# Two heads' last 64 keys turned and multiplied as one block, and a pair's outputs gathered in one bank

## The reference, cut to what matters

```python
# batch 4, 8 heads, 576 rows, 64 channels a head
scores = scale * np.matmul(q, k.transpose(0, 1, 3, 2))
thresh = np.max(scores, axis=-1, keepdims=True) - tau
scores = np.where(scores >= thresh, scores, -1000000000.0)
scores = scores - np.max(scores, axis=-1, keepdims=True)
attn = np.exp(scores)
attn = attn / (np.sum(attn, axis=-1, keepdims=True) + 1e-09)
attn_out = np.matmul(attn, v)
# then a gated layer on the heads side by side: k = relu(xk @ w_k), v = k*k @ w_v, times sigmoid(xr @ w_r);
# then a two-dimensional Fourier transform, a normalisation and relu(un @ w_ch1) @ w_ch2
```

## Time and profile before

| | us |
|---|---|
| median of 3 runs | 1071.75 (1071.11 to 1073.01) |
| profiled execution, device time | 1072.66 |
| its span | 1070.9 |
| PE busy in the span | 1051.8 |
| DVE busy | 577.4 |
| ACT busy | 513.3 |
| POOL busy | 414.1 |

### The profile page before, as it was taken

The page is one execution under the profiler, slowest core; times in us unless marked ns, Lnnn a source line. Parts: engine busy times, 40 slices in busy tenths (PEclk is TensorE's granted clock), DMA queues, the critical chain, the costliest instruction groups (busy, mean ns, idle before and its releaser), DMA issues.

```text
span 1070.9 us, 18505 instructions
## 1 busy us (share of the span) xinstructions
PE 1051.8 (98%) x7088; PEld 1000.9 (93%) x7088; DVE 577.4 (54%) x1119; ACT 513.3 (48%) x1252; POOL 414.1 (39%) x362
## 2 busy tenths in 40 slices
PE   7999899999999999999999999999999999999998
PEld 6999899999999999999999999888888888888998
DVE  6888885467965467865455788434214114123211
ACT  5999775646875646875746653121111111111110
POOL 4878784343664343664312345441111111111000
PEclk9999999999999999999999999999999999999999
DMA  8636111024211024211013217200100100100000
GB/s 242 192 89 194 36 49 49 11 80 126 87 41 56 4 80 126 94 34 36 2 45 142 79 50 289 96 1 36 36 1 27 45 1 8 63 2 1 36 1 34
DMA packets 39992, 70.10 MB, mean 65 GB/s; under 512 B 4320, under 2 KB 21088, under 8 KB 39392
## 3 DMA queue, kind: packets, MB, share of 16 engines
q1 hardware_dynamic: 39600, 68.59, 20.2%
q10 hardware_dynamic: 304, 0.33, 0.1%
HBM read 56.50 MB, written 12.41 MB: 64 GB/s over the span
## 4 chain that ended last, share of the span: by engine, by line
PE 89%; POOL 4%; ACT 3%; DVE 2%; issue 1%; DMA 0%; SPq 0%; DVEq 0%; ACTq 0%; POOLq 0%
PE PB L807 22%; PE PB L809 21%; PE PB L808 21%; PE PB L867 11%; PE PB L834 7%; PE PB L850 6%; ACT probsT L1121 1%; ACT exps L1112 1%; POOL wkl L673 1%; DVE probs L1392 1%; POOL cs_lo L685 0%; POOL k_lo L664 0%; DVE neg_s L1381 0%; POOL q_hl L657 0%; DMA k_raw<-kT_dram 0%
## 5 line engine op out<-in xcount | busy, mean ns | idle before, releaser
L1340 ACT ACTIVATE h_hi<-PB 128x464 fp32r<-128x464 f32 (+1 forms) x80 | 44.5, 556 | 329.8 <-PE PB L809 329.8
L1615 DVE SCALAR_TENSOR_TENSOR h_lo<-PB,h_hi 128x464 fp32r<-128x464 f32 (+1 forms) x80 | 51.0, 638 | 256.7 <-ACT h_hi L1340 256.7
L867 PE MATMUL PB<-v_sb,probsT 128*128 128x64 f32 (+1 forms) x1440 | 177.8, 271 | 0.0
L867 PEld LDWEIGHTS PB<-v_sb,probsT 128*128 128x128 f32 x1440 | 172.6, 192 | 0.0
L1392 DVE SCALAR_TENSOR_TENSOR probs<-neg_s,thresh,exps 128x576 f32<-128x576 f32 x144 | 160.0, 1111 | 2.7 <-ACT exps L1112 2.3
L1121 ACT ACTIVATE probsT<-PB 128x384 f32<-128x384 f32 (+1 forms) x288 | 110.6, 439 | 78.1 <-PE PB L850 77.0
L1381 DVE TENSOR_SCALAR_CACHE_REDUCE neg_s<-PB,taus 128x576 f32<-128x576 f32 x144 | 117.0, 813 | 47.9 <-PE PB L834 44.6
L809 PE MATMUL PB<-un_h,w1l 128*128 128x464 f32 (+1 forms) x320 | 118.8, 371 | 0.0
L808 PE MATMUL PB<-h_lo,w2h 128*128 128x464 f32 (+1 forms) x320 | 118.8, 371 | 0.0
L807 PE MATMUL PB<-h_hi,w2h 128*128 128x464 f32 (+1 forms) x320 | 118.8, 371 | 0.0
L809 PE MATMUL PB<-h_hi,w2l 128*128 128x464 f32 (+1 forms) x320 | 118.8, 371 | 0.0
(11 more groups left out here) (195 smaller groups left out, 2359.7 us busy)
## 6 DMA issues: line engine op xcount, KB each, us to landing
q_raw<-qT_dram SPq DMA_DIRECT2D x62, 160.0 KB, 3.1
k_raw<-kT_dram SPq DMA_DIRECT2D x64, 144.0 KB, 3.2
w_raw<-w_dram SPq DMA_DIRECT2D x8, 1024.0 KB, 8.2
u_scr<-x2T SPq DMA_DIRECT2D x4, 1152.0 KB, 4.8
cd<-cd_scr SPq DMA_DIRECT2D x4, 1032.0 KB, 4.9
v_sb<-v_dram SPq DMA_DIRECT2D x16, 256.0 KB, 3.1
u_in<-u_scr SPq DMA_DIRECT2D x4, 928.0 KB, 5.1
out_dram<-u_in SPq DMA_DIRECT2D x16, 232.0 KB, 2.2
```

The source lines that it names most:

```text
L867: last = nc.tensor.matmul(bank(6 + p)[:, i * DH:i * DH + width], probsT[:, n % 2, kt * P128:(kt + 1) * P128], v_sb[:, kt, pair % 2, p * DH ...
L1615: nc.vector.scalar_tensor_tensor(h_lo[:, ft % 3, 0:w], bank(4 + ft % 3)[:, 0:w], 0.0, h_hi[:, ft % 3, 0:w].bitcast(F32), ALU.max, ALU.subt ...
```

## The change

For a first head's tile the last 64 keys are not turned and not multiplied: they stay in `probs`. The second head's tiles now run in falling order of rows (`row_of`), so that tile 8 - jj of the second head meets tile jj of the first in the same one of the two buffers. `place_of` shifts each tile in its buffer so that the first head's last 64 keys end up right beside the second head's, and both are turned as one block of 128. The values' fifth block holds the second head's last 64 keys in rows 0 to 63 and the first head's in rows 64 to 127, with zeros elsewhere, and one matmul of 128 columns adds both heads' shares. So a pair's outputs for the same rows lie side by side, in bank 6 + pair % 2; those of tile 4 lie in the other of the two banks. In tile 4 a copy of the last 64 keys (`both_last`) is made by one more DVE instruction, so that its block of 128 is full too.

```diff
+def full_first(n):
+    return n % TILES_PAIR < TAIL
...
+def place_of(n):
+    return (2, 2, 1, 1, 0, 0, 0, 1, 1)[n % TILES_PAIR] * DH
...
 def units_of(n):
-    return [(2 * n, 0, 3), (2 * n + 1, 3, KT)]
+    some, all_of = (2, KT - 1) if full_first(n) else (3, KT)
+    return [(2 * n, 0, some), (2 * n + 1, some, all_of)]
...
-    return jj - QT if jj > TAIL else jj
+    return TILES_PAIR - 1 - jj if jj > TAIL else jj
...
+COPIED_AT = {0: (TAIL,), 2: (0, 1), 3: (2, 3)}
...
+        def outputs(pair, i):
+            at = 0 if i == TAIL else i * 2 * DH
+            return bank(6 + (pair + (i == TAIL)) % 2)[:, at:at + 2 * DH]
...
-                        sp.dma_start(v_sb[0:64, 4, pair % 2, :], v[b * S + 512:b * S + S, cols]).then_inc(v_in[pair % 2], 16)
+                        for h in range(2):
+                            rows = slice(DH * (1 - h), DH * (1 - h) + DH)
+                            sp.dma_start(v_sb[rows, 4, pair % 2, h * DH:h * DH + DH], ...
...
                         for kt in range(k0, k1):
...
+                            if kt == KT - 1 and n % TILES_PAIR == TAIL:
+                                keys = both_last[:, :, :].rearrange("p a n -> p (a n)")
+                            else:
+                                keys = probs[:, n % 2, at + kt * P128:at + (kt + 1) * P128]
...
-                    if jj in (0, QT) and n >= TILES_PAIR:
-                        pe.wait_ge(head_out, pair * 2 + p - 1)
+                    if pair > 0 and jj == 0:
+                        pe.wait_ge(tile_out, (pair - 1) * QT + 1)
+                    if pair > 0 and jj == TAIL:
+                        pe.wait_ge(tile_out, pair * QT)
...
-                    for kt in range(KT):
-                        last = nc.tensor.matmul(bank(6 + p)[:, i * DH:i * DH + width], ...
+                    for kt in range(KT - 1):
+                        last = nc.tensor.matmul(both[:, own], probsT[:, n % 2, kt * P128:(kt + 1) * P128], ...
+                    if jj >= TAIL:
+                        last = nc.tensor.matmul(both, probsT[:, n % 2, (KT - 1) * P128:KT * P128], v_sb[:, KT - 1, pair % 2, :], ...
...
-                        pe.wait_ge(head_out, d * H + 2 * dt + 2)
+                        pe.wait_ge(tile_out, (d * PAIRS + dt + 1) * QT)
...
-                    for again in (False, True):
-                        done = n - 4 - again
-                        if 0 <= done < TILES and done % TILES_PAIR in (TAIL, TILES_PAIR - 1):
-                            copy_head(done, again)
+                    pair, at = divmod(n - 10, TILES_PAIR)
+                    if 0 <= pair < B * PAIRS:
+                        for i in COPIED_AT.get(at, ()):
+                            copy_tile(pair, i)
...
+                    if jj == TAIL:
+                        twice = [t[:, n % 2, FULL * P128:S].unsqueeze(1).broadcast_to([P128, 2, DH]) for t in (neg_s, exps)]
+                        nc.vector.scalar_tensor_tensor(both_last[:, :, :], twice[0], thresh[:, col:col + 1], twice[1], ALU.is_le, ALU.mult)
...
-                            dve.wait_ge(head_out, head - 1)
+                            dve.wait_ge(tile_out, pair * QT)
```

More of the change, by code:

```diff
@@ L1129, in copy_head @@
                         if pair >= PAIRS:
                             act.wait_ge(tx_ready, pair // PAIRS * 5)
-                    col = pair % PAIRS * 2 * DH + p * DH
-                    some = (3, FULL) if p == 0 else (2, FULL)
-                    for i in range(some[0], some[1]) if again else range(some[0]):
-                        t = i + p * QT
-                        last = nc.scalar.activation(x_att[:, i, col:col + DH], bank(6 + p)[:, i * DH:(i + 1) * DH],
-                                                    ACT.Copy, scale=rowinv[:, t:t + 1])
@@ L1138, in copy_head @@
[L1138 to L1145 removed]
+                    else:
+                        act.wait_ge(pv_ready, (pair + 1) * TILES_PAIR)
+                        act.wait_ge(inv_ready, pair * 2 + 2)
@@ new lines, in copy_tile @@
+                    for h in range(2):
+                        cols = slice(col + h * DH, col + h * DH + DH)
+                        if i == TAIL:
+                            rows = slice(h * DH, h * DH + DH)
+                            last = nc.scalar.activation(x_att[0:DH, TAIL, cols], outputs(pair, i)[rows, h * DH:h * DH + DH], ACT.Copy, scale=rowinv[rows, TAIL:TAIL + 1])
+                        else:
+                            t = TILES_PAIR - 1 - i if h else i
+                            last = nc.scalar.activation(x_att[:, i, cols], outputs(pair, i)[:, h * DH:h * DH + DH], ACT.Copy, scale=rowinv[:, t:t + 1])
```

73 lines of the change are left out of this document (36 added, 37 removed).

## The result

| | before | after |
|---|---|---|
| median, us | 1071.57 (1071.11 to 1073.01) | 1061.35 (1060.88 to 1061.86) |
| profiled execution | 1072.66 | 1061.17 |
| its span | 1070.9 | 1059.4 |

The change made the kernel 10.2 us faster: the ratio is 0.9902, with a 95% interval of 0.9885 to 0.992. The forecast was 1058.0 with a range of 1053 to 1065. The sign and the range held. The size was 13.7 us by the sum; the two profiled executions show 11.5. That leaves 2.2 us to find in the trace.

The account below looks back on a forecast made before the run. PE's weight loads were taken to bound three stretches alone, with DVE and ACT limiting elsewhere. 12.2 + 2.5 + 0.7 - 1.2 - 0.5 = 13.7 us saved gave 1059.0 profiled, median 1058.0, range 1053 to 1065.

Parts of the forecast that it names:

- The prices: On PE, a turn costs 0.114 us, a matmul 0.222 to 0.224; widening the fifth turn and matmul costs nothing resolvable.
- The rival that priced a turn by its columns: On PE, a 64-column turn costs 0.057 us, so 5.2 us less is saved: 1063.2; chance 0.03.
- The three stretches, 12.2 us: Where PE's weight loads alone bound, first-head tiles of nine pairs save 1.35 us each, all of it taken.
- the pairs between them (+0.7): Pairs 8 and 12, paced by DVE and ACT in turn: one tile of four ahead saves, 2 x 0.34 us.
- the copies (-1.2): Ahead of a batch's last turn, extra output copies on ACT delay DVE and ACT 0.4 us in three batches.
- PE alone: PE bounds all along, DVE and ACT only follow it; all 21.6 us come, 1050.2; chance 0.07.
- the stretches fill up: DVE and ACT follow late in the full stretches, half the 12.2 us is lost: 1066.1; chance 0.07.
- The last batch's 0.5 us: Before the last batch's mixing, all four extra copies stand among ACT's mixes and cost 0.5 us.
- The first batch: Up to 134 us, five pairs hold 6.75 us, of which 2.5 is taken: 1.35 + 0.43 + about 0.7.
- DVE idles 0.63 us in this very slot for ACT, which hides it: On DVE, the added instruction, 0.4 us a pair by width, is hidden; uncovered it costs 6.4 us.
- The first pair's 1.35 comes through.: In the first batch, the first pair's whole PE saving of 1.35 us is won.
- The slower rival: DVE waits for ACT's late copies, closing a ring over every pair: 32 us against 21.6 saved, 1082.2; chance 0.03.

Follow-up runs that it names:

- the waits filled: Changed kernel with 12 idle turns on PE ahead of the last turn of `x_att` in batches 0, 1 and 2; median 1060.91 us.
- four copies fewer: Changed kernel without the first head's four full output copies of the last pair in batches 1 and 2; median 1060.54 us.
- no `both_last`: Changed kernel without the DVE instruction that makes `both_last`, tile 4's last 64 keys left out of the sum with the values; median 1060.54 us.

## Why the prediction was right, and what it missed

- **The prices** of turn, matmul and both widenings (0.11, 0.223, 0, 0) are in the trace of after to 0.01 us. The rival that priced a turn by its columns is refuted: the fifth turn takes 0.11 us at 128 columns, as at 64.
- **The three stretches, 12.2 us, with the pairs between them (+0.7) and the copies (-1.2)**: 11.7 us foreseen between marks 0 and 3, 10.5 measured, and 11.2 with the waits filled (157.1 + 160.0 + 158.9 less 153.1 + 156.5 + 155.2). Neither of the rivals "PE alone" and "the stretches fill up" came. But single terms are off by more than their sum. The last batch's 0.5 us did not show, and that this makes good for the 0.5 missing here is luck. The first scores of each tile (L834 before, L863 after) show it tile by tile:

| us saved at the first scores of tile | 9 | 18 | 27 | 36 | 54 | 63 | 72 | 81 |
|---|---|---|---|---|---|---|---|---|
| after | 1.49 | 0.45 | 0.95 | 1.15 | 2.80 | 4.03 | 5.27 | 5.13 |
| four copies fewer | 0.77 | -0.07 | 0.43 | 0.64 | 2.27 | 3.50 | 4.74 | 4.82 |
| no `both_last` | 2.85 | 1.97 | 3.34 | 2.10 | 4.43 | 5.65 | 6.89 | 5.51 |

Where PE alone bounds, a pair gives 1.24 us (tiles 54 to 63, 63 to 72), not 1.35. The pair between, tiles 72 to 81, gives 0.08 where the copies are left out, not 0.35. The copies cost 0.2 to 0.3 us a batch, not 0.4.

- **The first batch** gave 1.1 us up to mark 0 where 2.5 were taken. The step that failed is the one on DVE: "DVE idles 0.63 us in this very slot for ACT, which hides it". That row stood in the second batch. In the first, DVE of the changed kernel had no such idle time there, and two inputs beside POOL's two made 0.34 us into 0.48 to 1.49. The text put this at 6.4 us over 16 pairs if uncovered (ends 2.7 and 11.7), but priced it by width, and took it at nothing in the only batch where it was uncovered. Measured without it: mark 0 is 1.0 us earlier, mark 1 1.7.
- **A second step in the first batch**, which no run takes apart: "The first pair's 1.35 comes through." By the table most of what is saved at tile 9 is gone at tile 18, and without `both_last` 0.9 us of it go too. In that stretch ACT makes four output copies in each of two slots that follow each other, 0.94 and 0.99 us, where before made two, 0.55 and 0.58, and PE waits twice for the units behind them:

```profile
37.88 0.94 ACT L1177 ACTIVATE x_att<-PB,rowinv 128x64 f32<-128x64 f32 x4
40.98 0.99 ACT L1177 ACTIVATE x_att<-PB,rowinv 128x64 f32<-128x64 f32 x4
```
```profile
41.00 0.42 PEld L881 LDWEIGHTS PB<-ident,probs 128*128 128x128 f32 x4 [1.30 <-issue]
44.15 0.42 PEld L881 LDWEIGHTS PB<-ident,probs 128*128 128x128 f32 x4 [1.30 <-issue]
```

The forecast priced the late copies only ahead of a batch's last turn. That they cost in the first batch too is likely, not shown: no kernel spreads them out there.

- **PE's longer wait before the last turn** was foreseen in kind (0.35 to near 1 us) and became 1.48. By itself it costs nearly nothing: filled with idle turns or taken away, the slots around it stay as long. Its price came through the clock, 0.7 us in the profile; the medians say 0.4 (1061.35 against 1060.91). The forecast had no term for that.
- **The slower rival**, a ring through `tile_out`, was rightly given 0.03: no gap ahead of any sum, and relaxing the wait wins nothing. Only without `both_last` does this wait show.
- The missing 2.2 us are then 1.4 in the first batch, of which `both_last` explains 1.0 at mark 0, and 0.7 in the fall of the clock, while the errors of the other terms cancel.

What stays open: why a fall comes in one execution and not in the next of the same kernel, and why it lasts 3.4 us in one and 7 in another. Why a pair in a full stretch gives 1.24 us and not 1.35, though each turn and matmul has its price. And how much the bunched copies cost in the first batch.

## What to carry to other kernels

A saving on the engine that bounds comes through where it bounds alone; cut the program into stretches, and check each added instruction in the stretch where its engine has no slack, not in one where it happens to idle. Price a two-input DVE instruction beside a busy POOL by POOL's instructions (here up to 1.6 us for what takes 0.34 alone), not by its width. When less work leaves longer waits on PE, look at the granted clock in windows of 2 us; here a dozen idle turns in each such wait took 0.7 us out of the profile, and four executions then lay within 0.2 us.
